# Inverse squares of a running product: a suffix product on VectorE, or the logarithm and exponential of the product's own squares on ScalarE

## The reference

```python
mag = np.sqrt(a_re * a_re + a_im * a_im)
scale = np.minimum(mag, 0.999) / (mag + 1e-06)
a_re_n, a_im_n = (a_re * scale, a_im * scale)
for t in range(S):
    new_re = ar * S_re - ai * S_im
    new_im = ar * S_im + ai * S_re
    kv = np.einsum('bhd,bhe->bhde', k[:, :, t], v[:, :, t])
    S_re, S_im = (new_re + kv, new_im)
    y[:, :, t] = np.einsum('bhd,bhde->bhe', q[:, :, t], S_re)
```

## Time and profile before

| | us |
|---|---|
| median of 3 runs | 668.25 (667.24 to 670.85) |
| the profiled execution | 667.75 |
| its span in the trace | 666.0 |
| busy: TensorE, VectorE, ScalarE, POOL | 517.3, 418.1, 324.4, 147.8 |

### The profile page before, as it was taken

The page is one execution under the profiler, slowest core; times in us unless marked ns, Lnnn a source line. Parts: engine busy times, 40 slices in busy tenths (PEclk is TensorE's granted clock), DMA queues, the critical chain, the costliest instruction groups (busy, mean ns, idle before and its releaser), DMA issues.

```text
span 666.0 us, 11747 instructions
## 1 busy us (share of the span) xinstructions
PE 517.3 (78%) x4538; PEld 396.1 (59%) x4538; DVE 418.1 (63%) x680; ACT 324.4 (49%) x563; POOL 147.8 (22%) x128
## 2 busy tenths in 40 slices
PE   2000039796597977997887999989999999999996
PEld 1000016675375755775666874548888888888885
DVE  4799998979969999997734315167533333232331
ACT  5774135383455736332222332267665555565652
POOL 6001000100001000010000000036655555555653
PEclk9655569798797987998987999999999999999999
DMA  6400084724926434688698699900010101010101
GB/s 252 142 1 0 3 221 99 151 76 104 245 48 136 115 86 91 132 273 208 189 256 233 132 424 423 434 11 1 1 48 0 49 0 48 1 48 1 44 5 47
DMA packets 39558, 79.59 MB, mean 119 GB/s; under 512 B 7120, under 2 KB 28752, under 8 KB 37200
## 3 DMA queue, kind: packets, MB, share of 16 engines
q1 hardware_dynamic: 36192, 62.33, 33.1%
q10 hardware_dynamic: 3312, 16.52, 7.5%
HBM read 55.12 MB, written 4.72 MB: 90 GB/s over the span
## 4 chain that ended last, share of the span: by engine, by line
PE 53%; DVE 22%; DMA 9%; issue 6%; ACT 4%; SPq 4%; POOL 0%; ACTq 0%; DVEq 0%; POOLq 0%
PE ps L1248 10%; PE ps L1250 10%; PE ps L1249 10%; DMA stk<-xout 8%; PE ps L992 8%; SPq L253 4%; PE ps L1230 3%; DVE big L670 3%; DVE xout L791 2%; DVE tt L695 2%; DVE big L700 2%; PE ps L978 2%; PE ps L1150 2%; PE ps L1172 2%; DVE big L659 2%
## 5 line engine op out<-in xcount | busy, mean ns | idle before, releaser
L962 DVE TENSOR_TENSOR qs<-rs 128x512 f32<-128x512 f32 x96 | 75.1, 782 | 129.2 <-ACT rs L563 129.2
L626 POOL TENSOR_TENSOR hlo<-qs,hhi 128x512 fp32r<-128x512 f32 x96 | 126.9, 1322 | 125.4 <-DVE qs L962 122.0
L992 PE MATMUL ps<-stk 112*128 112x224 f32 (+1 forms) x384 | 94.3, 412 | 53.4 <-DMA stk<-xout 53.3
L978 PE MATMUL ps<-ident 128*32 128x512 bf16 x246 | 71.2, 391 | 69.0 <-DVE xout L791 69.0
L992 PEld LDWEIGHTS ps<-stk 112*128 112x128 f32 x384 | 83.2, 237 | 66.4 <-DMA stk<-xout 59.7
L1248 PE MATMUL ps<-hhi,who 128*128 128x512 f32 x288 | 112.1, 389 | 1.6 <-POOL hlo L626 1.6
L1250 PE MATMUL ps<-hhi,wlo 128*128 128x512 f32 x288 | 112.0, 389 | 0.0
L1249 PE MATMUL ps<-hlo,who 128*128 128x512 f32 x288 | 112.0, 389 | 0.0
L563 ACT ACTIVATE rs<-ps 128x512 f32<-128x512 f32 x96 | 57.5, 599 | 83.7 <-PE ps L1230 83.6
L978 PEld LDWEIGHTS ps<-ident 128*32 128x32 bf16 x246 | 19.3, 96 | 88.9 <-DVE xout L791 69.3
L613 POOL MEMSET big<- 128x2304 f32 x4 | 8.2, 2038 | 266.1 <-DVE big L700 266.1
(11 more groups left out here) (155 smaller groups left out, 811.3 us busy)
## 6 DMA issues: line engine op xcount, KB each, us to landing
stk<-xout SPq DMA_DIRECT2D x144, 128.0 KB, 3.6
wt<-in_w SPq DMA_DIRECT2D x10, 1536.0 KB, 12.3
xq<-in_xq SPq DMA_DIRECT2D x24, 384.0 KB, 4.3
wt<-in_w ACTq DMA_DIRECT2D x6, 1536.0 KB, 10.4
big<-in_a_all ACTq DMA_DIRECT2D x9, 768.0 KB, 4.8
vr<-in_v_all SPq DMA_DIRECT2D x24, 192.0 KB, 4.0
out<-ost SPq DMA_DIRECT2D x6, 768.0 KB, 3.5
wins<-in_w_in SPq DMA_DIRECT2D x1, 3072.0 KB, 17.4
```

Of the source, the lines that this page charges most:

```text
L626: pool.tensor_tensor(hlo[:, i % NHS, :], qs[:, i % NQS, :], hhi[:, i % NHS, :].bitcast(F32), ALU.subtract).then_inc(lo_ready, 1)
L962: dve.tensor_tensor(qs[:, i % NQS, :], rs[:, i % NQS, :], rs[:, i % NQS, :], ALU.mult).then_inc(sq_ready, 1)
L978: nc.tensor.matmul(ps[P - SL:P, bank, :], idb[:, 0:SL], idle, start=True, stop=True)
L992: last = nc.tensor.matmul(ps[:, h // 2, h % 2 * SK:h % 2 * SK + cols], x[:, 0:CH], x[:, CH:CH + cols], start=True, stop=True)
```

## The change

M_ is now taken from the products themselves: ScalarE squares the two planes of E_j (`product_squares`, into `M_` and the scratch `N_`), VectorE adds them (`square_sums`), ScalarE takes the logarithm and then the exponential of its negative (`inverse_squares`), in place. The first three of four blocks are one piece of 6 x 288 elements per partition, the last a second one of 6 x 96. The layout of `M_` becomes that of the planes, so `weigh` reads it in steps of two elements. `scaled_mag`, `norm_squares`, `end_norms`, `inverses` and POOL's two memsets per batch go. `key_query(n, 0)` stands ahead of `weigh(n)`. The shares of the parts change, and `turn_factors` becomes the last one; the wait of `stack_turns` is for its end as before.

```diff
@@ SyncE
-                sp.wait_ge(chain, C_ALL * b + C_TURN)
+                sp.wait_ge(chain, C_ALL * (b + 1))
@@ ScalarE
-            def norm_squares(b):
...
+            def product_squares(b, part):
+                act.wait_ge(chain, C_ALL * b + (C_BLOCK if part else C_BLOCK - 7))
+                if b >= 2 and part == 0:
+                    act.wait_ge(weighed, NC * (b - 1))
+                x, dims = PART[part]
+                e = PL[b % 2] + x
+                nc.scalar.activation(grid(M_[b % 2] + x, *dims), grid(e, *dims), ACT.Square).then_inc(m_squares, 1)
+                nc.scalar.activation(grid(N_ + x, *dims), grid(e + PF, *dims), ACT.Square).then_inc(m_squares, 1)
+
+            def inverse_squares(b):
+                for part in range(2):
+                    act.wait_ge(chain, C_ALL * b + C_BLOCK + part + 1)
+                    x, dims = PART[part]
+                    m = grid(M_[b % 2] + x, *dims)
+                    nc.scalar.activation(m, m, ACT.Ln).then_inc(m_log, 1)
+                act.wait_ge(m_log, 2 * (b + 1))
+                m = grid(M_[b % 2], [1, PF])
+                nc.scalar.activation(m, m, ACT.Exp, scale=-1.0).then_inc(m_ready, 1)
@@ ScalarE, the loop over stages p and chunks c
-                    if c == 0 and p < B:
-                        norm_squares(p)
+                    if c == NC - 1 and p < B:
+                        product_squares(p, 0)
...
+                    if c == NC - 1 and p < B:
+                        product_squares(p, 1)
...
+                    if c == NC - 1 and p < B:
+                        inverse_squares(p)
                     if c == NC - 1 and p < B - 1:
                         signs(p + 1)
@@ VectorE
+            def square_sums(b, part):
+                dve.wait_ge(m_squares, 4 * b + 2 * part + 2)
+                x, dims = PART[part]
+                m = grid(M_[b % 2] + x, *dims)
+                dve.tensor_tensor(m, m, grid(N_ + x, *dims), ALU.add).then_inc(chain, 1)
...
-                dve.wait_ge(chain, C_ALL * (b + 1))
+                dve.wait_ge(m_ready, b + 1)
...
-            parts = [4] + [14] * (BL - 1) + [48] * (NB4 - 1) + [8, 18, 52]
+            parts = [4] + [14] * (BL - 1) + [48] * (NB4 - 1) + [20, 9, 18]
...
-                        weigh(n)
                         key_query(n, 0)
+                        weigh(n)
                         key_query(n, 1)
```

More of the change, by code:

```diff
@@ L205, in program @@
         C_BLOCK = C_SCAN + 7 * (NB4 - 1)
-        C_END = C_BLOCK + 3
-        C_TURN = C_END + 10
-        C_ALL = C_TURN + 1
+        C_END = C_BLOCK + 2
+        C_ALL = C_END + 10
+        BC = BL * NC
+        PART = [(0, ([HP, TF], [1, (NB4 - 1) * BC])), ((NB4 - 1) * BC, ([HP, TF], [1, BC]))]
         def turns(n):
@@ L608, in _ @@
             assert made[0] == NCONST
[L610 to L615, removed]
             pool.wait_ge(y_done, NT)
@@ L737, in turn_factors @@
                 n1 = NC - 1
+                dve.wait_ge(chain, C_ALL * b + C_BLOCK)
                 if b:
@@ L762, in turn_factors @@
                 dve.tensor_tensor(gd[:, 1, :, :, 1], u1[:, 0], u2[:, 0], ALU.add).then_inc(chain, 1)
[L764 to L769, removed]
             def weigh(n):
                 b, c = divmod(n, NC)
-                dve.wait_ge(chain, C_ALL * (b + 1))
+                dve.wait_ge(m_ready, b + 1)
                 dve.wait_ge(ld_xq[n % NXQ], 16 * (n // NXQ + 1))
-                x = xq[:, n % NXQ, 1].rearrange("p t (f j) -> p (t f) j", f=2)
-                dve.tensor_tensor(x, x, grid(M_[b % 2] + HC * c, [HP, TF], [1, HC]), ALU.mult).then_inc(weighed, 1)
+                x = xq[:, n % NXQ, 1].rearrange("p t (j i) -> p t j i", i=2)
+                x = bass.AP(xq, x.offset, [list(xq[:].ap[0]), [HC, TF], [2, HC // 2], [1, 2]])
+                dve.tensor_tensor(x, x, grid(M_[b % 2] + 2 * c, [HP, TF], [2 * NC, HC // 2], [1, 2]), ALU.mult).then_inc(weighed, 1)
             def key_query(n, inverse):
@@ L782, in key_query @@
                     dve.wait_ge(weighed, n + 1)
-                elif n >= NOUT:
-                    k = n - NOUT
-                    dve.wait_ge(stacked[k % NST], 96 * (k // NST + 1))
+                else:
+                    dve.wait_ge(chain, C_ALL * (b + 1))
+                    dve.wait_ge(ld_xq[n % NXQ], 16 * (n // NXQ + 1))
+                    if n >= NOUT:
+                        k = n - NOUT
+                        dve.wait_ge(stacked[k % NST], 96 * (k // NST + 1))
                 e = grid(PL[b % 2] + 2 * c, [HP, 2 * TF], [2 * NC, HC // 2], [1, 2])
@@ L830, in part @@
                     block_step(b, k - BL + 1)
-                elif k == BL + NB4 - 1:
-                    end_norms(b)
-                elif k == BL + NB4:
+                elif k < BL + NB4 + 1:
+                    square_sums(b, k - BL - NB4 + 1)
+                else:
                     turn_factors(b)
-                else:
-                    inverses(b)
             def parts_in(b, lo, hi):
@@ L855, in _ @@
                 normalise(0, t)
-            for t in range(DT):
-                scaled_mag(0, t)
             dve.wait_ge(consts, NCONST)
@@ L887, in _ @@
                             norm2(p + 1, t)
-                    if p < B - 1 and c == NC - 1:
-                        for t in range(DT):
-                            scaled_mag(p + 1, t)
             running_max(NT // 2 - 1)
```

25 lines of the change are left out of this document (4 added, 21 removed).

## The result

| | before | after |
|---|---|---|
| median, us (range, runs) | 667.75 (666.8 to 670.85, 4) | 690.55 (686.81 to 691.85, 4) |
| profiled execution / its span | 667.75 / 666.0 | 689.56 / 687.8 |
| busy: TensorE, VectorE, ScalarE, POOL | 517.3, 418.1, 324.4, 147.8 | 514.9, 399.1, 351.7, 139.8 |

The change makes the kernel slower: 1.033 times the time before, interval 1.0289 to 1.0371. VectorE has 19 us less to do, and the span is 21.8 us longer.

A forecast was written before the change was run, and what follows sets the result against it. VectorE leads narrowly, but TensorE's wait for each batch's last-chunk stacks decides: leads of -6, about 0 and +7 after batches 0 to 2, +25.7 at chunk 18, +24.5 at the end, on 667.75 give 692 us; bounds 678 and 703.

The forecast's parts named there:

- A: End of ScalarE's copy of negated logits in chunk 4 of a batch; squares start behind it, exponential ends 11.3 us later.
- `weigh` in steps of two: VectorE's weighting reads its factors in steps of two elements; put at nothing, as neighbouring products do so at full rate.
- VectorE's wait ahead of the sums: VectorE waiting for ScalarE before the sum of 1728: about 3 us in batches 1 and 2, 9 to 10 in 3.
- copy's end to gst: From the end of the negated-logits copy to the end of the turn factors, when gst DMAs start: 7.1 us.
- about 0: Lead (new minus old time) at the end of batch 1, chunk 6: the 6 us gained earlier are gone.
- Lead after batch 0: New minus old time at the start of batch 1's products: -6, at 81.1 instead of 87.19 us.
- Contention in batch 1: Raw loads beside the last chunk's stack DMAs: 2 us added, between 0 and 4.
- Within batch 3 TensorE runs its chunks back to back in both cases and can't make it up: Lead of +7 us from batch 2 persists in batch 3, so its copy ends at 329.5 instead of 322.5.
- may come back: After chunk 18: a microsecond recovered from TensorE's earlier stack waits, 1.9 us before chunk 18 alone; lead +24.5.
- Rival 1: VectorE stays the bound, so the 5.7 us a batch come through: about 648 us; chance 5%.
- Rival 2: Only the last batch pays, TensorE's idle times at batch ends taking up part of the delay: 678 us; chance 20%.
- Rival 4: Squares at the strided rate and full contention of stacks with raw loads: about 703 us; chance 14%.

The follow-up runs named there:

- experiment 4: Changed kernel with the raw loads of batch 2 issued behind ScalarE's copies of chunk 5: 687.41 us, 1.029 of the kernel before.
- Experiments 7: Changed kernel with turn factors ahead of the sums, even shares, all squares behind chunk 4's key copies, exponential ahead of its last copies: 668.26 us, 0.998 of before.
- 8: Changed kernel with turn factors ahead of the sums, third block product last, all squares early (second pair behind the state copy): 668.67 us, 1.002 of before.
- experiment 12: Experiment 9's kernel with the three weight loads of stage 4 behind the key copies of chunks 18 to 20: 667.32 us, 1.000 of before.
- experiment 3: Kernel before the change with only its turn factors moved last, behind the scan: 679.22 us, 1.018 of before.
- 5: Changed kernel with only the first pair of squares moved up, behind chunk 4's key copies: 680.46 us, 1.018 of the kernel before.
- experiment 9: Kernel 8 with the last chunk's stack DMAs issued ahead of the gst DMAs: 672.02 us, 1.005 of the kernel before.
- experiment 6: Changed kernel with the last chunk's stack DMAs issued ahead of the gst DMAs in SyncE's queue: 680.43 us, 1.020 of the kernel before.

## Why the prediction was right

692 was forecast, 690.55 measured; the chain is the one foreseen. Point by point:

| step | predicted | measured |
|---|---|---|
| squares of 1728, both sums, exponential's end | 1.6; 2.5; A + 11.3 | 1.63; 2.63; A + 11.2 |
| `weigh` in steps of two | free | 551 ns, 547 before |
| VectorE's wait ahead of the sums | 3, 3, 9 to 10 | 3.04, 3.04, 8.85 |
| copy's end to gst | 7.1 | 7.0, 7.0, 7.0 |
| gst issues | 156.9, 249.3, 336.6 | 160.2, 253.8, 336.0 |
| scores of chunks 5, 11, 17 | 170.7, 260.5, 348.2 | 176.0, 264.7, 347.0 |
| scores of chunk 18 | 357.4 | 356.0 |
| idle ahead of 5, 11, 17 | 18 each | 22.3, 17.5, 17.5 |

The intermediate times of batches 1 and 2 are 3 to 5 us off, and the end is right to 1.5. The mechanism was foreseen; that the number is so close is partly luck. Two terms were too small for the delay and one too large (besides a lead of 1.2 us at chunk 6 that I rounded to "about 0"), and they cancelled:

- *Lead after batch 0, taken as -6.* VectorE's part held: products of batch 1 at 80.44 (81.1 forecast). But the stacks of chunk 0, though issued 6.9 us sooner (79.52 against 86.43), brought the scores only 4.0 sooner (94.04 against 98.00): 14.5 us instead of 11.6. The raw loads go out at 76.8, 78.3 and 79.9, the last behind the stacks' first issue (before, at 81.9, 83.5 and 85.2, all were ahead of it); I had counted such a meeting only at the end of batch 1. That it makes the 2.9 us is argued, no run takes it away. The lead at the copy of batch 1 was -2.7.
- *Contention in batch 1, taken as 2 between 0 and 4.* It was 4.7 (11.9 against 7.2, and experiment 4 takes it away). The rule of the Trainium skill, "DMA: Bandwidth & Descriptors", section "Queues, rings and completion order", that each DMA engine goes round its queues packet by packet, spoke for the whole 4, and the measurement sides with it; I should have gone by it.
- *"Within batch 3 TensorE runs its chunks back to back in both cases and can't make it up".* This is the step that failed, and it was wrong of the kernel before already:

```profile
310.26 4.91 PE L992 MATMUL ps<-stk 112*128 112x224 f32 x16 [4.33 <-DMA stk<-xout]
...
343.09 4.98 PE L992 MATMUL ps<-stk 112*128 112x224 f32 x16 [2.32 <-DMA stk<-xout]
```

  The delay was 13.1 us at the start of chunk 12 (274.75 against 261.62); 2.0 went with its warm start (I had 1.5), which leaves 11.1 at chunk 13. Then TensorE's wait ahead of chunk 16 shrank from 4.33 to 1.78 us, and this chunk too ran its scores in 3.29 instead of 4.91, since the idle stretch ahead was short. With that the copy ends 6.4 us late and not, as I had it, 7 from a delay of 7. TensorE had slack in that batch, and a late TensorE finds its stacks ready.

Behind chunk 18, +24.3 us became +21.8 in the span. The 2.5 recovered come at chunk 19: the wait ahead of it fell from 2.32 (second row above) to 1.40 us and its scores ran in 3.29 instead of 4.98. The 1.9 us ahead of chunk 18, of which I said "may come back", can't be among them: that wait ends before the scores of chunk 18 from which I counted.

Rival 1 (VectorE the bound, 648) is refuted by the result. Experiments 7, 8 and 12 speak against it too, since they are level, but the wait for the exponential is left in them, so what VectorE's saving is worth without any new wait stays open. Rival 2 (only the last batch pays) fails by the idle times ahead of chunks 5 and 11, though its reason, catching up, acted in batch 3. Rival 4 fails by the squares' 1.63 us, while its full contention came about. How the loss is split: place of the turn factors some 12 us (experiment 3), the wait for ScalarE the other 10 (5 gives them back); one chain, two halves.

Open: what in the even shares makes TensorE idle ahead of chunk 14, how bandwidth is shared in detail between large loads and stacks, what the kernel before gains from both edits of 12, and what experiment 12 would do with its exponential ready for chunk 18, which wasn't tried. That its 5.21 us are what keeps it level is argued from one row only.

## What to carry to other kernels

Before moving work to an idle engine, look at what stands ahead of it in that engine's queue: 11 us of ScalarE's work a batch, put behind a copy paced by TensorE, and small results for a third queue, put behind that work, together cost 22 us. An engine that is busy nine tenths of the time need not be worth its saving: with the queues mended as far as here, 5.7 us less a batch on VectorE bought nothing, and the wait that was left stood on the same path. And of a DMA that goes out at another time, ask what it then meets; at chunk 5 of the changed kernel and at chunk 18 of six versions it met a large load and lost 4 to 5 us. A version and its control must both be looked at for that.

## What the runs showed of the hardware

- Six stack DMAs of 128 KB took 7.1 to 7.7 us from first issue to scores by themselves. With three loads of 768 KB issued 1 to 4 us behind their start on another queue they took 11.9 (after), with one of 1.5 MB 1 to 3 us behind 11.6 to 12.4 (the table of experiment 9). So two very different loads cost about the same 4.7 us.
- A table load didn't wait with its activation. At the end of batch 0, where the logarithm waits for VectorE's sum, ScalarE had begun to load its table 3.2 us before and was done 1.9 us before:

```profile
67.03 1.28 ACT L376 ACT_TABLE_LOAD   x1
...
70.23 2.22 ACT L376 ACTIVATE big<-big 128x1728 f32<-128x1728 f32 x2 [1.92 <-DVE big L726]
```

  So of two loads of 1.28 us a batch, one can hide in the wait. The forecast of the exponential's end counted both, and in batches 1 to 3, where there is no such wait, both were paid.
- TensorE's granted clock was 0.66 in the mean from 330 to 360 us, where it idles 17.5 us for chunk 17: a mix of its two levels, 1.2 GHz (0.50) and 2.4 GHz (1.00). From 347 to 350 us, during that chunk's scores, it was 0.50, and they took 3.78 us. In experiment 6, with 1.5 us of idle time ahead, it was 1.00 from 323 to 325 us, and the same scores took 2.05. The window of the changed kernel:

```profile
330.00:360.00 30.00, 12.81 (x104) 10.54 (x105) 12.71 (x24) 13.42 (x18) 0.00 (x0) 0.66 0.62 132
```
